# Block decays by a tree of products: six levels summed on TensorE, or one level summed and five multiplied on VectorE

## The reference

```python
mag = sqrt(a_re^2 + a_im^2); scale = minimum(mag, 0.999) / (mag + 1e-6)
for t in range(S):
    S_re, S_im = ar*S_re - ai*S_im + outer(k[t], v[t]), ar*S_im + ai*S_re
    y[t] = q[t] @ S_re
x = y as (3072 tokens, 384)
x = relu(x @ w_in)^2 @ w_out              # d_ff 2048
out = (silu(x @ w_gate) * (x @ w_val)) @ w_out2   # d_ff 1536
```

## Time and profile before

| | |
|---|---|
| median of three runs | 1336.56 us |
| the profiled execution, own time | 1338.41 us |
| its span | 1336.6 us |
| granted clock, mean | 0.953 |
| TensorE (PE) busy | 1237.6 us, 93% |
| ScalarE (ACT) busy | 758.8 us, 57% |
| VectorE (DVE) busy | 740.7 us, 55% |
| GpSimd (POOL) busy | 158.7 us, 12% |
| chain that ended last | PE 73%, DVE 10%, ACT 10%, issue 6% |

### The profile page before, as it was taken

One profiled execution on the slowest core, in us unless ns is written; L12 is line 12 of the kernel. 1 busy time (PEld: TensorE's weight loads), 2 busy tenths in 40 slices (PEclk: granted clock), 3 DMA queues, 4 the chain that ended last, 5 costly groups with the idle time before them and its releaser, 6 DMA issues.

```text
span 1336.6 us, 26664 instructions
## 1 busy us (share of the span) xinstructions
PE 1237.6 (93%) x10390; PEld 1158.2 (87%) x10390; DVE 740.7 (55%) x1204; ACT 758.8 (57%) x1473; POOL 158.7 (12%) x140
## 2 busy tenths in 40 slices
PE   2666899999998998998999998999999999999998
PEld 2554788888888887888888898999999999999998
DVE  4888777777777777777777740134322222222322
ACT  5666778787887887887887844652222222222221
POOL 1000122122122121121221222300000000000000
PEclk9556899999999999999999997999999999999999
DMA  3321111111111111111211102240101001000000
GB/s 134 111 88 54 36 37 55 59 45 55 54 37 55 54 37 55 54 38 54 59 50 37 47 23 86 72 130 19 36 1 37 18 19 35 0 35 1 18 19 18
DMA packets 42139, 62.57 MB, mean 47 GB/s; under 512 B 3120, under 2 KB 37680, under 8 KB 41648
## 3 DMA queue, kind: packets, MB, share of 16 engines
q1 hardware_dynamic: 42032, 60.99, 14.6%
HBM read 46.83 MB, written 14.16 MB: 46 GB/s over the span
## 4 chain that ended last, share of the span: by engine, by line
PE 73%; DVE 10%; ACT 10%; issue 6%; ACTq 0%; DVEq 0%
PE bank L1334 7%; PE bank L1332 7%; PE bank L1333 7%; PE bank L1240 5%; PE bank L1241 4%; PE bank L1242 4%; PE bank L1355 4%; PE bank L1351 4%; PE bank L1353 4%; PE bank L1253 4%; PE bank L1257 3%; PE bank L1255 3%; PE bank L1173 3%; PE bank L1229 2%; PE bank L1119 2%
## 5 line engine op out<-in xcount | busy, mean ns | idle before, releaser
L442 POOL TENSOR_TENSOR glo<-rg,ghi 128x384 fp32r<-128x384 f32 x128 | 153.6, 1200 | 712.1 <-ACT ghi L607 712.1
L1069 DVE TENSOR_TENSOR prod<-bank,silu 128x384 f32<-128x384 f32 x96 | 53.5, 557 | 285.4 <-PE bank L1334 269.1
L715 ACT ACTIVATE silu<-bank 128x384 f32<-128x384 f32 x84 | 41.4, 493 | 281.0 <-PE bank L1334 281.0
L1240 PE MATMUL bank<-xhi,win_hi 128*128 128x384 f32 x384 | 141.4, 368 | 8.0 <-DVE xlo L961 6.5
L1253 PE MATMUL bank<-ghi,wout_hi 128*128 128x384 f32 x384 | 135.3, 352 | 0.0
L1241 PE MATMUL bank<-xlo,win_hi 128*128 128x384 f32 x384 | 133.0, 346 | 0.0
L1242 PE MATMUL bank<-xhi,win_lo 128*128 128x384 f32 x384 | 132.9, 346 | 0.0
L1257 PE MATMUL bank<-ghi,wout_lo 128*128 128x384 f32 x384 | 129.4, 337 | 0.0
L1255 PE MATMUL bank<-glo,wout_hi 128*128 128x384 f32 x384 | 129.0, 336 | 0.0
L1173 PEld LDWEIGHTS bank<-QT,KT 112*64 112x64 f32 x2304 | 79.1, 147 | 48.2 <-issue 26.9
L1173 PE MATMUL bank<-QT,KT 112*64 112x64 f32 x2304 | 89.4, 235 | 30.5 <-issue 12.8
(11 more groups left out here) (161 smaller groups left out, 3045.6 us busy)
## 6 DMA issues: line engine op xcount, KB each, us to landing
gates_sb<-in_gates SPq DMA_DIRECT2D x48, 192.0 KB, 2.4
qk_sb<-in_qk SPq DMA_DIRECT2D x24, 384.0 KB, 3.1
v_sb<-in_v SPq DMA_DIRECT2D x24, 192.0 KB, 3.2
xT_scratch<-yT SPq DMA_DIRECT2D x48, 96.0 KB, 2.0
xin<-xT_scratch SPq DMA_DIRECT2D x8, 576.0 KB, 4.0
y1T_scratch<-y1s SPq DMA_DIRECT2D x8, 576.0 KB, 3.5
x<-y1T_scratch SPq DMA_DIRECT2D x8, 576.0 KB, 4.0
out<-o_sb SPq DMA_DIRECT2D x8, 576.0 KB, 3.0
```

What stands on the lines that cost most here:

```text
L442: pool.tensor_tensor(glo[:, j % GR, :], rg[:, j % 2, :], ghi[:, j % GR, :].bitcast(F32), ALU.subtract)\
L1240: nc.tensor.matmul(banks[4][:, 0:UT], win_hi[:, k, c], xhi[:, k, :], start=k == 0, stop=False)
```

## The change: what it does

`spans` becomes `halves`, the 32 blocks of 4 steps alone. `Dn` has 32 rows, `DT` 8 x 16 blocks of two halves (256 elements a partition). The decays of the longer blocks are no longer sums of logarithms, but products on VectorE: `T8` is the product of the two halves of each block of 8, `T16` that of pairs of `T8`, and so on to `T128`, the decay of the chunk. `tree8` takes the place and the waits of `at_free`. `T16` and `T32` are made behind `in_block`, `T64` and `T128` behind `neighbours16`. The scalings read `DT` and the `T` tiles in three dimensions instead of four. ScalarE's copy into `DT` waits for `t8` of the chunk before instead of `sdec`.

```diff
-SPANS = (4, 8, 16, 32, 64, 128)
-ND = 64
...
-    spans = np.concatenate([s // L == np.arange(CH // L)[None, :] for L in SPANS], axis=1)
-    spans = np.pad(spans, ((0, 0), (0, ND - spans.shape[1])))
+    halves = s // mid == np.arange(CH // mid)[None, :]
...
+    NH8 = CH // BLK
...
-        Dn = A("Dn", [ND, H, P])
+        Dn = A("Dn", [2 * NH8, H, P])
...
-        DT = A("DT", [KR, H, ND])
+        DT = A("DT", [KR, H * NH8, 2])
+        T8, T16 = A("T8", [KR, H * NH8]), A("T16", [KR, H * NH8 // 2])
+        T32, T64, T128 = A("T32", [KR, H * 4]), A("T64", [KR, H * 2]), A("T128", [KR, H])
...
-                act.wait_ge(ev["sdec"], n - 1)
-                act.activation(DT[:, :, :], banks[0][0:KR, :].rearrange("p (h c) -> p h c", h=H),
+                act.wait_ge(ev["t8"], n - 1)
+                act.activation(DT[:, :, :], banks[0][0:KR, 0:2 * H * NH8].rearrange("p (b r) -> p b r", r=2),
                                ACT.Copy).then_inc(ev["DTev"], 1)
...
             def decay_state(n):
+                dve.wait_ge(ev["t128"], n)
                 dve.wait_ge(ev["pY"], n)
                 dve.tensor_tensor(St[:, :, :], St[:, :, :],
-                                  bc(span(CH), [KR, H, D]), ALU.mult)\
+                                  bc(T128[:, :].rearrange("p (h a) -> p h a", a=1), [KR, H, D]), ALU.mult)\
...
+            def tree8(n):
+                dve.wait_ge(ev["pY"], n - 1)
+                dve.wait_ge(ev["p0"], n)
+                dve.tensor_tensor(T8[:, :], DT[:, :, 0], DT[:, :, 1], ALU.mult).then_inc(ev["t8"], 1)
+
+            def tree(n, dst, src, ready, done):
+                x = src[:, :].rearrange("p (b r) -> p b r", r=2)
+                dve.wait_ge(ready, n)
+                dve.tensor_tensor(dst[:, :], x[:, :, 0], x[:, :, 1], ALU.mult).then_inc(done, 1)
...
-            def at_free(n):
-                dve.wait_ge(ev["pY"], n - 1)
-                dve.wait_ge(ev["p0"], n)
-                dve.memset(Dn[0:1, 0, P - 1:P], 0.0).then_inc(ev["atf"], 1)
...
             def to_borders16(n):
+                dve.wait_ge(ev["t8"], n)
...
                 for x, own in ((QT, 1), (KT, 0)):
-                    a, d = own_other(x, 8, own)
+                    a, d = own_other(x, T8, 8, own)
...
-                    at_free(n)
+                    tree8(n)
                     in_block(n)
+                    tree(n, T16, T8, ev["t8"], ev["t16"])
+                    tree(n, T32, T16, ev["t16"], ev["t32"])
...
                     neighbours16(n)
+                    tree(n, T64, T32, ev["t32"], ev["t64"])
+                    tree(n, T128, T64, ev["t64"], ev["t128"])
                     to_borders64(n)
...
                 for h in range(H):
-                    ins = nc.tensor.transpose(banks[0][0:KR, h * ND:(h + 1) * ND], Dn[:, h, 0:KR], ident[0:ND, 0:ND])
+                    ins = nc.tensor.transpose(banks[0][0:KR, h * 2 * NH8:(h + 1) * 2 * NH8], Dn[:, h, 0:KR],
+                                              ident[0:2 * NH8, 0:2 * NH8])
```

More of the change, by code:

```diff
@@ L58, in constant_tables @@
     suffix = s > t
-    spans = np.concatenate([s // L == np.arange(CH // L)[None, :] for L in SPANS], axis=1)
-    spans = np.pad(spans, ((0, 0), (0, ND - spans.shape[1])))
-    f = [x.astype(np.float32) for x in (np.eye(CH), run_sum, last_row, around_mid, suffix, spans)]
+    halves = s // mid == np.arange(CH // mid)[None, :]
+    f = [x.astype(np.float32) for x in (np.eye(CH), run_sum, last_row, around_mid, suffix, halves)]
     mats = np.concatenate(f, axis=1)
@@ L132, in build @@
             lrhi lrlo thhi thlo cyhi cylo r32
-            pQT pKT pDT QTev KTev DTev p0 atf sc8 m0 p8 sc16 m8 p16 sc32 m16 p32 sc64 c32
+            pQT pKT pDT QTev KTev DTev t8 t16 t32 t64 t128 p0 sc8 m0 p8 sc16 m8 p16 sc32 m16 p32 sc64 c32
             p64 scF c64 pY yev pS sdec sadd"""
@@ L240, in build, with own_other @@
         NAT = lambda i: banks[i][:, 0:HD]
-        def span(L):
-            i = sum(CH // x for x in SPANS if x < L)
-            return DT[:, :, i:i + CH // L]
-        def span_of(L, r, n):
-            x = span(L).rearrange("p h (b r) -> p h b r", r=2)[:, :, :, r:r + 1]
-            return bc(x, [KR, H, CH // (2 * L), n])
-        def own_other(x, L, own):
-            x5 = x[:, :, :].rearrange("p h (b r e) -> p h b r e", r=2, e=L)[:, :, :, own, :]
-            return x5, span_of(L, 1 - own, L)
+        def own_other(x, T, L, own):
+            nb = H * CH // (2 * L)
+            x4 = x[:, :, :].rearrange("p h (b r e) -> p (h b) r e", r=2, e=L)[:, :, own, :]
+            return x4, bc(T[:, :].rearrange("p (b r) -> p b r", r=2)[:, :, 1 - own:2 - own], [KR, nb, L])
         def half_views(r, bank):
@@ L522, in block_decays @@
                 act.wait_ge(ev["pDT"], n - 1)
-                d_in = banks[1][0:ND, 0:HD].rearrange("p (h d) -> p h d", h=H)
+                d_in = banks[1][0:2 * NH8, 0:HD].rearrange("p (h d) -> p h d", h=H)
                 for r in range(2):
@@ L883, in to_borders @@
                 for x, x0, r in ((QT, QT0, 0), (KT, KT0, 1)):
-                    x4, x04 = (y[:, :, :].rearrange("p h (b e) -> p h b e", e=BLK) for y in (x, x0))
-                    dve.tensor_tensor(x4, x04, span_of(BLK // 2, r, BLK), ALU.mult).then_inc(ev["sc8"], 1)
-            def at_free(n):
-                dve.wait_ge(ev["pY"], n - 1)
-                dve.wait_ge(ev["p0"], n)
-                dve.memset(Dn[0:1, 0, P - 1:P], 0.0).then_inc(ev["atf"], 1)
+                    x3, x03 = (y[:, :, :].rearrange("p h (b e) -> p (h b) e", e=BLK) for y in (x, x0))
+                    dve.tensor_tensor(x3, x03, bc(DT[:, :, r:r + 1], [KR, H * NH8, BLK]), ALU.mult)\
+                        .then_inc(ev["sc8"], 1)
             def in_block(n):
@@ L913, in to_borders32 @@
             def to_borders32(n):
+                dve.wait_ge(ev["t16"], n)
                 dve.wait_ge(ev["sc16"], 2 * n)
@@ L917, in to_borders32 @@
                 for x, own in ((QT, 1), (KT, 0)):
-                    a, d = own_other(x, 16, own)
+                    a, d = own_other(x, T16, 16, own)
                     dve.tensor_tensor(a, a, d, ALU.mult).then_inc(ev["sc32"], 1)
@@ L925, in to_borders64 @@
             def to_borders64(n):
+                dve.wait_ge(ev["t32"], n)
                 dve.wait_ge(ev["sc32"], 2 * n)
@@ L928, in to_borders64 @@
                 for x, own in ((QT, 1), (KT, 0)):
-                    a, d = own_other(x, 32, own)
+                    a, d = own_other(x, T32, 32, own)
                     dve.tensor_tensor(a, a, d, ALU.mult).then_inc(ev["sc64"], 1)
             def to_start(n):
+                dve.wait_ge(ev["t64"], n)
                 dve.wait_ge(ev["sc64"], 2 * n)
                 dve.wait_ge(ev["p64"], n)
-                a, d = own_other(QT, 64, 1)
+                a, d = own_other(QT, T64, 64, 1)
                 dve.tensor_tensor(a, a, d, ALU.mult).then_inc(ev["scF"], 1)
```

4 lines of the change are left out of this document (2 added, 2 removed).

## The result

The change makes the kernel slower by half a per cent. Twenty runs gave a median of 1340.68 us (1338.69 to 1348.63), twenty runs of the kernel before on the same chips 1335.88 us (1330.2 to 1343.28). The ratio is 1.0051 [1.0036, 1.0066]: +6.8 us by the ratio, +4.8 us by the medians. Two repeats of the changed kernel gave 1.0071 [1.005, 1.0092] and 1.0052 [1.0032, 1.0072], and two repeats of the kernel before against itself 1.0016 [0.999, 1.0043] and 1.0017 [0.9992, 1.0041]. The forecast was 1346.4 us, +9.85 us on the span, with 1333 to 1357 as range. The sign held; the size was too large by three to five us.

The account below looks back on a forecast made before the run. TensorE was taken to bound the steady attention phase (536 of 560 us busy), VectorE unit 0. Terms 1.65 + 5.6 + 2.4 - 0.1 - 0.4 - 0.1 + 0.8 gave +9.85 us on 1336.56: 1346.4 us, range 1333 to 1357.

Parts of the forecast that it names:

- The second chunks: Second chunks, units 1 to 7: T8 held by GpSimd; +0.65 us at scores32, +0.15 at scores64; 7 x 0.8 = +5.6.
- The third chunks: Third chunks, units 1 to 6: T64 and T128 push L930's QT past GpSimd's start; 6 x 0.4 = +2.4 us.
- First chunks without a turn: Units 2 and 7 meet GpSimd like second chunks, +0.4 us each; unit 1's first waits for TensorE as well, -0.1.
- bare length: Rival from the experiments' theory: the cost is the five products' length wherever they stand; no chance given.
- Unit 0: Three chunks without GpSimd: +0.55 us each before L907, shorter DT copy hidden, 0.28 fits L930's wait; +1.65 us.
- Loop turns: Four first chunks behind a loop turn: waits swallow the products, 0.1 us of transposes gained each; -0.4 us.
- the transposes: TensorE's eight transposes of Dn move 32 columns instead of 64: 0.1 us saved a chunk, between 0 and 0.2.
- Swallowed: Rival: VectorE's idle time and L801's wait absorb most of the products; +2 us, 1338.5 us; chance 0.3.
- Faster: Rival: savings reach scores32 and L919's QT falls behind the GpSimd product; -6 to -8 us, 1329; chance 0.1.
- All of it: Rival: neither ScalarE's waits nor loop turns cover anything; 24 x 0.83 = +20 us, 1356 us; chance 0.12.
- The clock: Rival: longer gaps in unit 0 keep TensorE at 1.2 GHz longer; two microseconds more within range; no chance given.
- the rival of the repeat's expectation: Repeat of products in waits: a cost remains outside units 1 to 7, in unit 0; ratio repeats at 1.003.

Follow-up runs that it names:

- all products in waits: Changed kernel with memset back, T8 behind in_block, T16 and T32 behind to_borders16, T64 and T128 behind to_borders64 from unit 1: 1340.07 us, ratio 1.0033.
- the repeat: The kernel with all products moved into VectorE's waits, measured once more, unchanged, against the kernel before: 1339.41 us, ratio 1.0015.
- With the bank: Changed kernel with T8 at its place reading one input from the PSUM bank from unit 1, other four products in VectorE's waits: 1338.97 us, ratio 1.0027.
- T8 behind the mask: Changed kernel with T8 moved behind in_block (the masked copy) and the memset back in front: 1337.73 us, ratio 1.0035 to the kernel before.
- T8 from the bank: Changed kernel with T8 in its place, from unit 1 reading one input from the PSUM bank instead of DT: 1337.21 us, ratio 1.002.
- T64 and T128 late: Changed kernel with T64 and T128 made behind to_borders64 in the units that have MLP work: 1340.35 us, ratio 1.0046.
- the run with the cost alone: Kernel before, keeping its sums, plus the five products at the change's places, results unused: 1347.71 us, ratio 1.0111.

## Why the prediction was right in its sign and too high in its size

**The second chunks** (+5.6 forecast, +5.7 measured). T8 is held for 0.61 us more than its own 0.29; L801's wait swallows its 1.04 us; the scalings move through GpSimd's subtractions, one hold goes (L919's QT) and two come (L907's QT, L785). `capped` (L768) comes 1.13 us later in the chunk, where 1.1 was forecast, and the last KT 0.62 (0.65). What lies between was read wrong: I had expected L907 and the former L794 to give part back by moving into the subtractions. L907's hold gives nothing back, it costs 0.83 us and uses up most of L801's wait; and L785's 0.82 stands in for the 0.82 that L919's QT loses. That the 0.65 came out although these two were misread is partly luck.

The Trainium skill ("SBUF — State Buffer", section on the two separate sides of SBUF) says that GpSimd and a VectorE instruction with two SBUF inputs exclude each other for a whole instruction, whoever starts first. The pair 0.90 and 0.29 us for the same T8 agrees with it.

**The third chunks** (+2.4 forecast, +1.75 measured). The mechanism is the forecast one, 0.29 instead of 0.4 a chunk; undoing it took the chunk back to 32.06.

**First chunks without a turn** (+0.8 forecast for units 2 and 7, +0.67 measured; -0.1 forecast for unit 1, +0.53 measured). The step that failed is "the first of unit 1 waits for TensorE as well". VectorE does wait for it, 1.67 us at 140.10, but only behind `scores32`. From `to_borders` on VectorE works without a gap up to the last KT for `scores32`, before and after (a few rows, first before):

```profile
128.61 1.22 DVE L885 TENSOR_TENSOR KT<-KT,DT 112x1024 f32<-112x1024 f32 x1
...
129.77 0.06 DVE L891 MEMSET Dn<- 1x1 f32 x1
...
136.81 0.68 DVE L919 TENSOR_TENSOR KT<-KT,DT 112x512 f32<-112x512 f32 x1
```

```profile
126.43 1.22 DVE L889 TENSOR_TENSOR KT<-KT,DT 112x1024 f32<-112x1024 f32 x1
127.57 0.28 DVE L875 TENSOR_TENSOR T<-DT 112x128 f32<-112x128 f32 x1
...
135.18 0.68 DVE L920 TENSOR_TENSOR KT<-KT,T 112x512 f32<-112x512 f32 x1
```

The chunk begins at 125.95 before and 123.77 after. KT of `to_borders` begins 2.66 us into it in both, the last KT for `scores32` 10.86 and 11.41: the bare length of T8, T16 and T32, 0.55 us, comes through to `scores32` and stays to the chunk's end as +0.53. GpSimd has no part in it: it has no instruction here before 147.68 (146.00 after), T8 takes its own 0.28 us, and reading it from the bank changes nothing. I had carried the picture of the earlier trace rows over to a chunk that I had not looked at. So in this kind of chunk the rival "bare length" is the true one.

The 16 chunks come to +8.6 us where the terms gave 8.7 (5.6 + 2.4 - 0.1 + 0.8), since this miss and the smaller price of the third chunks cancel: that the total is right is luck in this part.

**Unit 0** (+1.65 forecast, -0.5 measured in the mean of three). The step "+0.55 us before L907 reaches `scores16` and `scores32`" failed. The third chunk is the clean one, 30.35 us in all three executions before and 30.39 in the one after that is shown. VectorE there, first before (the chunk begins at 95.60):

```profile
96.93 1.22 DVE L885 TENSOR_TENSOR QT<-QT,DT 112x1024 f32<-112x1024 f32 x1 [1.92 <-ACT DT L556]
...
106.51 0.69 DVE L907 TENSOR_TENSOR QT<-QT,DT 112x512 f32<-112x512 f32 x1
...
110.32 0.69 DVE L919 TENSOR_TENSOR QT<-QT,DT 112x512 f32<-112x512 f32 x1 [0.46 <-issue]
```

and after (from 93.38):

```profile
94.46 1.22 DVE L889 TENSOR_TENSOR QT<-QT,DT 112x1024 f32<-112x1024 f32 x1
...
104.57 0.69 DVE L907 TENSOR_TENSOR QT<-QT,T 112x512 f32<-112x512 f32 x1
...
108.11 0.69 DVE L920 TENSOR_TENSOR QT<-QT,T 112x512 f32<-112x512 f32 x1 [0.20 <-PE bank L1181]
```

Two things take the products in. VectorE does wait for DT here, against the text of the prediction, and the first scaling begins 0.25 us earlier in the chunk (1.08 instead of 1.33), so L907 comes only 0.28 us later and not 0.55. And I had used the 0.30 us in front of L930 and overlooked that L919 waits too, 0.46 us; that wait falls to 0.20 and L920 begins where L919 did (14.73 and 14.72 us into the chunk). The rest goes into L930's, which is 0.29 us before and gone after. Of 0.83 us of products 0.04 remained.

The other two chunks of unit 0 differ between executions of the kernel before, the second by 2.3 us: 32.55, 30.68 and 33.01 at granted clocks of 0.56, 0.67 and 0.59. In the changed kernel all three chunks repeat within 0.04 us (31.69 to 31.70 for the second, at 0.57 each time). So the -0.5 is the changed kernel's steady 95.4 against a mean of 94.5, 96.2 and 96.8.

**Loop turns** (-0.4 forecast, -2.7 measured in the mean of three). That the products are swallowed there was right. The step that failed is that the stop itself stays the same: the four stops summed to 12.8, 12.0 and 11.6 us in the three executions before and to 9.0, 8.7 and 10.1 after. (They were not all over 3 us before, as the prediction reads the earlier trace rows: the first of them was 2.30 us.) This is the largest error of the sum, 2.3 us; unit 0's is 2.15. Whether the change does it or chance stays open (below): the three sums after lie under all three before, but each kernel has three of them, and among the other kernels with the products they run from 8.7 to 14.3 us.

**Prices.** The small products were estimated at 0.28, 0.22, 0.18, 0.16 and 0.16 us and took 0.28, 0.23, 0.19, 0.18 and 0.17; T8 held took 0.90 and not 1.1. The copy of DT takes 395 ns (378 forecast). The term mis-sized is the transposes: eight of them with 32 moving columns take 0.55 us start to start (from the 679.45 above to TensorE's next row, below), against 0.59 with 64.

```profile
680.00 0.44 PE L1248 MATMUL bank<-xhi,win_hi 128*128 128x384 f32 x1
```

That is 0.04 us a chunk and not 0.1: below 64 columns the time hardly falls. The waits for L920's and L932's KT rose, by PEld's rows from 16.7 to 21.8 us and by PE's from 6.4 (3.3 and 3.1) to 9.6, 8.3 us together (8 forecast). PEld's and PE's waits are for the same event, so this is no sum of lost time, only of rows.

**The rivals.** "Swallowed" was true of unit 0 and of the loop turns, not of the others. "Faster" fell with the second chunks: L920's QT came 1.45 us later in the chunk than L919's and was free, but L785 in front of it had taken the hold, as the text said against it. "All of it" (+20 us) fell in the sum; only the first chunk of unit 1 let the length of three products through. The clock had no part in the steady stretch (0.99 in both).

**What stays open.** Two kernels whose 16 chunks nearly equal those of before (all products in waits, with and without the bank) read 1.0015 to 1.0033 against it, 2 to 4 us. The kernel before reads 1.0016 and 1.0017 against itself in the same two series, so about half of that, if any, is theirs, and each of these intervals is about 0.2% wide to either side. Without the bank a part is in unit 0 and is no chance: it takes 97.12 us in both profiled executions, its third chunk 32.70 and 32.71 us at a granted clock of 0.55, where the kernel before has 30.35 at 0.66. That is the rival of the repeat's expectation, in the chunks if not in the ratio. With the bank unit 0 takes 94.8 us, so it doesn't explain that kernel. The loop turns and what is behind the last chunk differ by 3 us and more from execution to execution, and the runs don't divide the rest.

## What to carry to other kernels

Before an instruction is exchanged for another of almost the same length, look at what the old one passed: here a memset and a copy with one operand in a bank passed a busy GpSimd, and a product of two SBUF tiles in the same place took three times its own length. New VectorE work belongs where VectorE waits anyway, and if it can't go there, an operand in a bank took the hold off it here (in the chunk lengths: the gain in the whole time is near the noise). For the forecast, look at every kind of chunk once by itself, and list all waits along the path instead of the one nearest to the new work.

## What the runs showed of the hardware

**Stops at a loop turn come in two sizes.** At each of the four turns TensorE stops in front of `scores_mid` with no releaser. Beside the shorter stops (1.9 to 2.8 us) the trace has one packet of the instruction queue in flight at a time (once two that overlap by 0.06 us), beside the long ones (3.3 to 3.9 us) two. Two turns of one execution (third profile of the changed kernel), with the instruction queue's share of the stretches 515 to 520 and 615 to 618.5 us behind each (packets, MB, share of 16 engines):

```profile
519.89 1.98 PE L1181 MATMUL bank<-QT,KT 112*64 112x64 f32 x32 [3.73 <-issue]
...
q8 instruction: 2, 0.03, 5.2%
...
618.09 1.37 PE L1181 MATMUL bank<-QT,KT 112*64 112x64 f32 x32 [1.90 <-issue]
...
q8 instruction: 1, 0.02, 1.7%
```

The two packets of the first turn overlapped and took 4.2 us together (5.2% of 16 engines for 5 us), the one of the second 0.95 us. Four turns of 1.5 us difference are 6 us, as much as the whole effect measured here. Of the 56 turns in the fourteen profiled executions 25 are long. The changed kernel has one in twelve, T8 behind the mask and T8 from the bank none in eight, the kernel before seven in twelve, and with T64 and T128 late all four are long. What brings the second packet was not found.

**Who is next beside GpSimd.** A subtraction that has waited since the middle of a VectorE instruction goes ahead of VectorE's next one, even when that one follows without a gap: KT of L930 directly behind its QT was held, and T8, 0.12 us behind the end of KT, too. And it is not only products of two tiles: L785, which reads one SBUF tile, took 1.17 us instead of 0.35 beside the subtraction.

**Small VectorE products.** From 8 to 128 elements they take 0.17 to 0.29 us: about 0.16 us for the instruction and 1 ns an element. A tree that halves its width saves almost nothing from its third level on.

**The clock in unit 0.** The third chunk of unit 0 took 30.35 us before, and 33.02 in the run with the cost alone, with the same number of matmuls. Length, busy us, then PEclk of that chunk, first before, then in the run with the cost alone:

```profile
95.60:125.95 30.35, 19.09 (x227) 15.37 (x226) 24.54 (x40) 20.55 (x37) 0.00 (x0) 0.66 0.22 71
```

```profile
96.91:129.93 33.02, 23.38 (x227) 19.81 (x227) 26.88 (x47) 20.68 (x36) 0.00 (x0) 0.51 0.26 75
```

At 0.51 TensorE is at its 1.2 GHz level all along and needs 4.3 us more for the same work; 2.7 of them showed in the chunk. Whether the later scalings kept it there or this execution would have had it anyway, one profile doesn't tell; but the kernel with all products in waits shows the like twice, 32.70 and 32.71 us at 0.55.
